# Windowed attention with two gated layers on one core: value loads moved one sequence earlier in the load queue

## The chip, the cores and the metric

The kernel runs on one core of a Trainium2 chip. The metric is the time of the whole program on the device in microseconds (us); three runs of the kernel before gave 895.91, 896.13 and 896.91, a median of 896.13. Lower is better.

## The reference, cut to what matters

The program computes attention in a sliding window of 64 positions (4 batches, 8 heads, 576 positions, head size 64), and feeds its output, 2304 tokens of 512 values, to two layers:

```python
scores = scale * np.matmul(q, k.transpose(0, 1, 3, 2))
mask = (rel >= 0) & (rel < 64)                      # rel = query position - key position
attn = softmax(np.where(mask, scores, -1e9))
x = np.matmul(attn, v)                              # -> (2304, 512)
xn = x / sqrt(mean(x * x) + 1e-6) * rms_g           # layer 1
x = (silu(xn @ w_gate) * (xn @ w_val)) @ w_out      # d_ff 1536
x = square(maximum(x @ w_in, 0)) @ w_out2           # layer 2, d_ff 2048
```

All inputs and outputs are float32.

## The kernel before, in words

Two heads of one batch form a "sequence" of the kernel: there are 16 of them (SEQS), each with 9 blocks of 64 queries. The two heads lie in the two halves of the 128 partitions. q of a sequence is loaded into a block-diagonal tile, `q_diag`, by two transfers of 144 KB (one for each head, L357 and L358); k by one transfer of 288 KB into `k_sb` (L353); v by two transfers of 256 KB, `v_odd` and `v_even` (both L365). All of these are issued by SyncE (SP) on one queue, except three for the first sequence that ScalarE issues at the start (k of sequence 0, and the second head's q of it in two parts). q, k and v each have three buffers (QR, VR).

Four blocks form a group; 36 groups cover the 144 blocks, and a group can straddle two sequences. Every compute engine walks through slots `g` in an order written out by hand. In slot g TensorE computes the scores of group g (L611; where a sequence begins, a matmul with a mask, L606, comes first), then transposes the probabilities of group g-4 (L619), then multiplies the probabilities of group g-5 with v (L631). VectorE picks the window and takes maximum and sum (L1165 to L1180), ScalarE takes the exponential (L936) and copies out of PSUM, GpSimd (POOL) divides and masks (L506, L512). TensorE waits for q and k of a sequence where its first block stands in a group, and for v there five slots later. The first block of sequence s is block 9s, so it stands in group 9s // 4: groups 0, 2, 4, 6, 9, 11, 13, 15, 18, 20, 22 and so on.

The first group's inputs have a semaphore of their own, `first_in` (three transfers: k of sequence 0 and the q of its first four blocks for both heads). SP waits for it before it loads q of sequence 1.

A later load waits for its buffer to come free. q and k of sequence i wait until the scores of the last group that holds blocks of sequence i-3 are done (`qk_done`); v of sequence i waits until the v product of the last group of sequence i-3 is done (`pv_done`). `last_group(s)` is (9s+8)//4: 2, 4, 6, 8, 11, 13, 15 and so on. SP issues its transfers strictly in program order, so a wait for one buffer also holds back everything behind it. Within the loop SP also loads the first weights of layer 1: `load_w` behind the loads of iterations 3 and 5, `load_d` behind those of 8 and 9.

After slot 35 the attention part runs out, mixed with the normalisation of the first tokens and the first products of layer 1; from about 103 us on the two layers run with TensorE as the main engine. Nothing there is touched.

Of the kernel before, what the change touches and what calls it, by code (L numbers as in the profile page):

```python
# [52 lines left out]
SEQS = KT * BATCH  # L53
# [8 lines left out]
QR = 3  # L62
# [4 lines left out]
def last_group(seq):  # L67

    return (seq * NBLK + NBLK - 1) // GU
# [55 lines left out]
def build(nc, qT, kT, v_odd_in, v_even_in, w_gate, w_val, w_out, gains, w_in, w_down, outT):  # L125
    with ExitStack() as ctx:
# [132 lines left out]
        def first_layer(r):  # L259
            return r < PAIRS  # L260

        def tok(r):
            return r % PAIRS * PW
# [12 lines left out]
        def half_cols(r, k, c):  # L276

            return acts[:, k * TOKENS + tok(r) + c * NT:k * TOKENS + tok(r) + (c + 1) * NT]
# [5 lines left out]
        def two(t):  # L284
            return t.rearrange("p (k t) -> p k t", k=2)
# [17 lines left out]
        def steps_done(u):  # L303

            return u + 1 - PLAIN
# [11 lines left out]
        def raw_part(u, n, count=1):  # L317
            return w_raw[u % 2][:, n * HALF_K:(n + count) * HALF_K]
# [18 lines left out]
        def first_rows(row, part):  # L337

            return qT[bass.ds(row, HD), :].rearrange("d (b c) -> d b c", c=WIN)[:, part, :]
# [4 lines left out]
        @block.sync  # L344
        def _(sp):
            def q_rows(row):
                return qT[bass.ds(row, HD), :].rearrange("d (b c) -> d b c", c=WIN)

            def load_k(i):
                par = i % QR  # L350
                if i >= QR:
                    sp.wait_ge(qk_done, last_group(i - QR) + 1)
                sp.dma_start(k_sb[par][:], kT[bass.ds(i * P, P), :]).then_inc(qk_in[par], 16)  # L353

            def load_q(i):
                par = i % QR
                sp.dma_start(q_diag[par][0:WIN, :, 0:WIN], q_rows(i * P)).then_inc(qk_in[par], 16)  # L357
                sp.dma_start(q_diag[par][WIN:P, :, WIN:P], q_rows(i * P + HD)).then_inc(qk_in[par], 16)  # L358

            def load_v(i):  # L360
                n = i % VR
                if i >= VR:
                    sp.wait_ge(pv_done, last_group(i - VR) + 1)
                for dst, src in ((v_odd[n], v_odd_in), (v_even[n], v_even_in)):
                    sp.dma_start(dst[:].rearrange("p m c -> p (m c)"), src[bass.ds(i * P, P), :]).then_inc(v_in[n], 16)  # L365

            def load_w(u):

                if u >= 2:
                    sp.wait_ge(lo1_done, u - 1)  # L370
                    if u - 2 >= PLAIN:
                        sp.wait_ge(s_add, 4 * steps_done(u - 2))
                r = max(n for n in range(RUNS) if U0[n] <= u)
                s = u - U0[r]
                one, two_ = ((w_gate, s), (w_val, s)) if first_layer(r) else ((w_in, 2 * s), (w_in, 2 * s + 1))
                rows = [w.rearrange("(k p) f -> p k f", p=P)[:, :, n * P:(n + 1) * P] for w, n in (one, two_)]
                sp.dma_start(raw_part(u, RAW_A11, 2).rearrange("p (k f) -> p k f", k=KT),
                             rows[0]).then_inc(w_raw_in[u % 2], 16)
                sp.dma_start(two(raw_part(u, RAW_A21)), rows[1][:, 0:2, :]).then_inc(w_raw_in[u % 2], 16)
                if u >= 2:  # L380
                    sp.wait_ge(lo2_done, u - 1)
                sp.dma_start(two(raw_part(u, RAW_A22)), rows[1][:, 2:4, :]).then_inc(w_a22_in[u % 2], 16)

            def load_d(m):

                if m >= 2:
                    sp.wait_ge(dlo_done, m - 1)
                r = max(n for n in range(RUNS) if M0[n] <= m)
                src = w_out if first_layer(r) else w_down
                n = m - M0[r]  # L390
                sp.dma_start(d_raw[m % 2][:], src[n * P:(n + 1) * P, :]).then_inc(d_in_sem[m % 2], 16)

            def store(r, c):
                for k in range(KT):
                    if k % 2 == 0:
                        sp.wait_ge(evac_act, 4 * r + 2 * c + k // 2 + 1)
                    else:
                        sp.wait_ge(evac_dve, 4 * r + 2 * c + k // 2 + 1)
                    to = tok(r) + c * NT
                    sp.dma_start(outT[k * P:(k + 1) * P, to:to + NT], half_cols(r, k, c)).then_inc(stored, 16)  # L400

            sp.dma_start(q_diag[0][0:WIN, 0:GU, 0:WIN], first_rows(0, slice(0, GU))).then_inc(first_in, 16)
            sp.dma_start(q_diag[0][0:WIN, GU:NBLK, 0:WIN], first_rows(0, slice(GU, NBLK))).then_inc(qk_in[0], 16)
            load_k(1)
            sp.wait_ge(first_in, 48)
            load_q(1)
            load_k(2)
            load_q(2)
            load_v(0)
            sp.dma_start(gain[:], gains).then_inc(gain_in, 16)  # L410
            for i in range(SEQS):
                if i + QR < SEQS:
                    load_k(i + QR)
                    load_q(i + QR)
                if i + 1 < SEQS:
                    load_v(i + 1)
                if i in (3, 5):
                    load_w((i - 3) // 2)
                if i in (8, 9):
                    load_d(i - 8)  # L420

            for r in range(RUNS):
                for u in range(U0[r] + (2 if r == 0 else 3), U0[r + 1] + 2):
                    if u < U0[RUNS]:
                        load_w(u)
                for m in range(M0[r] + 2, M0[r + 1] + 2):
                    if m < M0[RUNS]:
                        load_d(m)
                if r + 1 < RUNS:
                    load_w(U0[r + 1] + 2)  # L430
                if not first_layer(r):
                    store(r, 0)
                    store(r, 1)
            sp.wait_ge(stored, 16 * 2 * KT * PAIRS)
# [963 lines left out]
```

## Time and profile before

| what | us |
|---|---|
| median of 3 runs | 896.13 |
| the profiled execution, its own time | 895.91 |
| its span, from first to last instruction | 894.2 |
| TensorE busy in the span | 883.4 |
| POOL busy | 576.1 |
| VectorE busy | 562.1 |
| ScalarE busy | 482.0 |

The execution's own time is 1.7 us more than its span. The kernel has two parts of unlike nature: attention in the first tenth, in which the transfers run nearly all of the time, and the two layers in the rest, in which they run about a fifth of it. The change touches loads of the first part alone.

### The profile page before, as it was taken

The page shows a single profiled execution, that of the slowest core. Times are in us where ns is not written, and L with a number is a line of the kernel's source. Part 1 is how long each engine was busy: PE and PEld are TensorE (multiplying, and loading weights), DVE is VectorE, ACT ScalarE, POOL GpSimd, SP SyncE. Part 2 cuts the span into 40 slices and gives each one's busy share as a digit, 9 for nine tenths or more (in the row PEclk, how much of TensorE's full clock was granted, in tenths as well). Part 3 has the DMA queues.
Part 4 walks back from the last instruction along what each step waited for, and adds up shares of the span by engine and source line. Part 5 has one row for each costly group of instructions (what it writes and reads, how often), then busy time and mean ns, then how long its engine had stood idle before and what let it go on. Part 6 is the DMA issues. An engine that isn't in the chain of part 4 may idle for free.

```text
span 894.2 us, 14547 instructions
## 1 busy us (share of the span) xinstructions
PE 883.4 (99%) x5356; PEld 879.4 (98%) x5356; DVE 562.1 (63%) x735; ACT 482.0 (54%) x848; POOL 576.1 (64%) x539
## 2 busy tenths in 40 slices
PE   7999999999999999999999999999999999999998
PEld 6999999999999999999999999999999999999998
DVE  7687658557757647855556767677377675577222
ACT  3897765635466654455554455544355544455332
POOL 7897579755379757368867368473387653585332
PEclk9999999999999999999999999999999999999999
DMA  9995222112222212222221222222422122420122
GB/s 226 260 254 139 61 71 72 57 57 71 73 75 71 72 54 59 83 66 74 74 72 50 82 63 77 61 60 71 141 78 72 54 61 70 147 71 27 51 71 95
DMA packets 105974, 76.97 MB, mean 86 GB/s; under 512 B 24496, under 2 KB 89008, under 8 KB 105904
## 3 DMA queue, kind: packets, MB, share of 16 engines
q1 hardware_dynamic: 105152, 75.60, 30.6%
q8 instruction: 43, 0.70, 0.4%
q10 hardware_dynamic: 752, 0.44, 0.2%
q14 instruction: 27, 0.22, 0.1%
HBM read 71.31 MB, written 4.72 MB: 85 GB/s over the span
## 4 chain that ended last, share of the span: by engine, by line
PE 94%; POOL 2%; ACT 1%; DVE 1%; issue 0%; DMA 0%; ACTq 0%; POOLq 0%; DVEq 0%
PE bank L656 29%; PE bank L658 29%; PE bank L657 29%; PE bank L611 2%; PE bank L631 2%; POOL wide L512 1%; PE bank L619 1%; POOL probs L506 1%; POOL sq L521 0%; ACT acts L854 0%; PE bank L650 0%; PE bank L641 0%; DMA q_diag<-in_qT 0%; ACT probsT L854 0%; DVE acts L1122 0%
## 5 line engine op out<-in xcount | busy, mean ns | idle before, releaser
L656 PE MATMUL bank<-xc_hi,w_hi 128*128 128x384 f32 x844 | 282.7, 335 | 0.0
L658 PE MATMUL bank<-xc_hi,w_lo 128*128 128x384 f32 x844 | 282.0, 334 | 0.0
L657 PE MATMUL bank<-xc_lo,w_hi 128*128 128x384 f32 x844 | 281.9, 334 | 0.0
L554 POOL TENSOR_TENSOR d_lo<-d_raw,d_hi 128x512 fp32r<-128x512 f32 x84 | 127.3, 1516 | 174.5 <-ACT d_hi L854 174.5
L656 PE MATMUL bank<-hs_hi,d_hi 128*128 128x384 f32 x672 | 225.1, 335 | 0.1
L658 PE MATMUL bank<-hs_hi,d_lo 128*128 128x384 f32 x672 | 224.5, 334 | 0.0
L657 PE MATMUL bank<-hs_lo,d_hi 128*128 128x384 f32 x672 | 224.5, 334 | 0.0
L1255 DVE TENSOR_TENSOR hs_lo<-h,hs_hi 128x768 fp32r<-128x768 f32 x84 | 86.4, 1029 | 137.1 <-ACT hs_hi L854 136.9
L657 PEld LDWEIGHTS bank<-xc_lo,w_hi 128*128 128x128 f32 x844 | 158.5, 188 | 0.0
L656 PEld LDWEIGHTS bank<-xc_hi,w_hi 128*128 128x128 f32 x844 | 158.5, 188 | 0.0
L658 PEld LDWEIGHTS bank<-xc_hi,w_lo 128*128 128x128 f32 x844 | 158.4, 188 | 0.0
L854 ACT ACTIVATE hs_hi<-h 128x768 fp32r<-128x768 f32 x84 | 70.8, 843 | 138.7 <-PE bank L658 138.7
L1099 DVE TENSOR_TENSOR w_lo<-w_raw,w_hi 128x1024 fp32r<-128x1024 f32 (+1 forms) x60 | 82.1, 1368 | 82.2 <-ACT w_hi L854 81.9
L656 PEld LDWEIGHTS bank<-hs_hi,d_hi 128*128 128x128 f32 x672 | 126.1, 188 | 1.4 <-issue 0.7
L657 PEld LDWEIGHTS bank<-hs_lo,d_hi 128*128 128x128 f32 x672 | 126.1, 188 | 0.0
L658 PEld LDWEIGHTS bank<-hs_hi,d_lo 128*128 128x128 f32 x672 | 126.1, 188 | 0.0
L854 ACT ACTIVATE w_hi<-w_raw 128x1024 fp32r<-128x1024 f32 (+1 forms) x120 | 111.7, 931 | 0.0
L478 POOL TENSOR_TENSOR w_raw<-w_raw 128x256 f32<-128x256 f32 x58 | 64.3, 1108 | 40.9 <-DMA w_raw<-in_w_val 22.7
L1108 DVE TENSOR_TENSOR w_lo<-w_raw,w_hi 128x768 fp32r<-128x768 f32 (+1 forms) x60 | 72.8, 1213 | 0.0
L547 POOL TENSOR_TENSOR h<-sbb,vb 128x384 f32<-128x384 f32 x34 | 55.7, 1637 | 25.1 <-ACT sbb L979 25.0
L985 ACT ACTIVATE sa<-ga 128x384 f32<-128x384 f32 x58 | 30.5, 526 | 66.0 <-DVE ga L1276 65.8
L854 ACT ACTIVATE c_t<-bank 128x384 f32<-128x384 f32 x58 | 28.5, 492 | 65.3 <-PE bank L658 65.3
(90 smaller groups left out, 1199.3 us busy)
## 6 DMA issues: line engine op xcount, KB each, us to landing
d_raw<-in_w_down SPq DMA_DIRECT2D x48, 256.0 KB, 2.6
w_raw<-in_w_gate SPq DMA_DIRECT2D x36, 256.0 KB, 2.9
w_raw<-in_w_val SPq DMA_DIRECT2D x72, 128.0 KB, 2.8
d_raw<-in_w_out SPq DMA_DIRECT2D x36, 256.0 KB, 2.6
w_raw<-in_w_in SPq DMA_DIRECT2D x24, 256.0 KB, 2.7
w_raw<-in_w_in SPq DMA_DIRECT2D x48, 128.0 KB, 2.5
out_T<-acts SPq DMA_DIRECT2D x24, 192.0 KB, 3.0
k_sb<-in_kT SPq DMA_DIRECT2D x15, 288.0 KB, 4.7
```

The source lines that it names most:

```text
L478: nc.gpsimd.tensor_tensor(raw_part(u, RAW_S3), raw_part(u, RAW_A11), raw_part(u, RAW_A21), ALU.subtract).then_inc(s_add, 1)
L547: nc.gpsimd.tensor_tensor(h_half(n, 1), sbuf_b[:], vb[:], ALU.mult).then_inc(hb_done, 1)
L554: nc.gpsimd.tensor_tensor(d_lo[m % 2][:], d_raw[m % 2][:], d_hi[m % 2][:].bitcast(F32), ALU.subtract).then_inc(dlo_done, 1)
L611: mm = pe.matmul(ps, q_diag[par][:, b, :], keys, start=b > 0, stop=True)
L656: pe.matmul(ps, w_h, v_h, start=first, stop=False, skip_group_check=joined)
L657: pe.matmul(ps, w_h, v_l, start=False, stop=False, skip_group_check=joined)
L658: return pe.matmul(ps, w_l, v_h, start=False, stop=last, skip_group_check=joined)
L854: nc.scalar.activation(to, of, ACT.Copy).then_inc(done, 1)
L985: nc.scalar.activation(sa[:], ga[:], ACT.Silu if first_layer(r) else ACT.Relu).then_inc(act_a_done, 1)
L1099: nc.vector.tensor_tensor(w_lo[u % 2][:, to], w_raw[u % 2][:, of], w_hi[u % 2][:, to].bitcast(F32), ALU.subtract).then_inc(lo1_done, 1)
L1108: nc.vector.tensor_tensor(w_lo[u % 2][:, to], w_raw[u % 2][:, of], w_hi[u % 2][:, to].bitcast(F32), ALU.subtract).then_inc(lo2_done, 1)
L1255: nc.vector.tensor_tensor(hs_lo[m % 2][:], h_chunk(r, m - M0[r]), hs_hi[m % 2][:].bitcast(F32), ALU.subtract).then_inc(hlo_done, 1)
```

## The change

In the prologue the k load of sequence 1 is issued behind the wait for `first_in` instead of ahead of it; v of sequence 1 is loaded right behind v of sequence 0, and q and k of sequence 2 come behind both. In the loop, iteration i loads v of sequence i+2 where it loaded v of sequence i+1. The k and q loads of one sequence, two helper functions before, are one. The same transfers are made as before.

```diff
-            def load_k(i):
+            def load_qk(i):
                 par = i % QR
                 if i >= QR:
                     sp.wait_ge(qk_done, last_group(i - QR) + 1)
                 sp.dma_start(k_sb[par][:], kT[bass.ds(i * P, P), :]).then_inc(qk_in[par], 16)
-
-            def load_q(i):
-                par = i % QR
                 sp.dma_start(q_diag[par][0:WIN, :, 0:WIN], q_rows(i * P)).then_inc(qk_in[par], 16)
                 sp.dma_start(q_diag[par][WIN:P, :, WIN:P], q_rows(i * P + HD)).then_inc(qk_in[par], 16)
...
-            load_k(1)
             sp.wait_ge(first_in, 48)
-            load_q(1)
-            load_k(2)
-            load_q(2)
+            load_qk(1)
             load_v(0)
+            load_v(1)
+            load_qk(2)
             sp.dma_start(gain[:], gains).then_inc(gain_in, 16)
             for i in range(SEQS):
                 if i + QR < SEQS:
-                    load_k(i + QR)
-                    load_q(i + QR)
-                if i + 1 < SEQS:
-                    load_v(i + 1)
+                    load_qk(i + QR)
+                if i + 2 < SEQS:
+                    load_v(i + 2)
                 if i in (3, 5):
                     load_w((i - 3) // 2)
                 if i in (8, 9):
```

## Rows read from the trace of the kernel before

**Rows 1.** Windows: stretch, us, busy time (count) of each engine, granted clock, DMA share, GB/s
```profile
12.00:66.00 54.00, 53.92 (x482) 53.23 (x482) 41.06 (x127) 45.29 (x117) 47.68 (x54) 1.00 1.16 261
66.00:103.00 37.00, 35.10 (x287) 34.16 (x286) 24.32 (x62) 30.36 (x71) 30.14 (x32) 1.00 0.44 116
103.00:894.00 791.00, 788.09 (x4558) 786.44 (x4556) 488.64 (x529) 403.92 (x659) 490.96 (x426) 1.00 0.24 71
```
**Rows 2.** Waits, 0 to 13 us: waiter <- awaited: us in total, times, longest us
```profile
PE bank L606 <- DMA q_diag<-in_qT: 4.7, 1, 4.7
PEld bank L606 <- DMA q_diag<-in_qT: 0.3, 1, 0.3
```
**Rows 3.** Waits, 13 to 46 us, the longest in total
```profile
DVE bank L1165 <- PE bank L611: 8.9, 13, 0.8
```
**Rows 4.** Timeline of SP, 0 to 21 us: start us, us, queue, line, what is issued
```profile
2.25 0.61 SPq L353 DMA_DIRECT2D k_sb<-in_kT  x1
...
4.67 0.55 SPq L357 DMA_DIRECT2D q_diag<-in_qT  x1
5.25 0.64 SPq L358 DMA_DIRECT2D q_diag<-in_qT  x1
...
7.86 0.62 SPq L365 DMA_DIRECT2D v_odd<-in_v_odd  x1
8.52 0.43 SPq L365 DMA_DIRECT2D v_even<-in_v_even  x1
...
20.50 0.33 SPq L365 DMA_DIRECT2D v_odd<-in_v_odd  x1
```
**Rows 5.** Timeline of TensorE: where sequences 1, 2, 5, 7, 9 begin (L606), two v products
```profile
8.96 0.23 PE L606 MATMUL bank<-first_mask,ident_bf 128*128 128x128 bf16 x1
...
12.27 0.22 PE L606 MATMUL bank<-first_mask,ident_bf 128*128 128x128 bf16 x1
...
27.30 0.22 PE L606 MATMUL bank<-first_mask,ident_bf 128*128 128x128 bf16 x1
...
29.19 0.39 PE L631 MATMUL bank<-probsT,v_odd 128*128 128x128 f32 x2
...
36.86 0.22 PE L606 MATMUL bank<-first_mask,ident_bf 128*128 128x128 bf16 x1
...
40.52 0.39 PE L631 MATMUL bank<-probsT,v_even 128*128 128x128 f32 x2
...
47.75 0.22 PE L606 MATMUL bank<-first_mask,ident_bf 128*128 128x128 bf16 x1
```
**Rows 6.** Line L358 (second half of q), the issues at 5.25 and 7.18 us
```profile
L358 SPq DMA_DIRECT2D q_diag<-in_qT x2: 635/636/637, 5.3 to 7.2; - x2
...
DMA to landing us min/median/max: 3.7/4.2/4.8
```
**Rows 7.** Line L365 (v), the issues at 7.86 and 8.52 us
```profile
L365 SPq DMA_DIRECT2D v_even<-in_v_even x1: 432/432/432, 8.5 to 8.5; - x1
...
DMA to landing us min/median/max: 4.5/4.6/4.7
```
**Rows 8.** Line L358, the issues at 10.90 and 13.97 us
```profile
L358 SPq DMA_DIRECT2D q_diag<-in_qT x2: 635/635/635, 10.9 to 14.0; - x2
...
DMA to landing us min/median/max: 5.2/5.7/6.2
```
**Rows 9.** Line L358, the issues at 22.41 and 29.24 us
```profile
L358 SPq DMA_DIRECT2D q_diag<-in_qT x2: 637/1134/1631, 22.4 to 29.2; - x2
...
DMA to landing us min/median/max: 6.5/6.8/7.1
```
**Rows 10.** Line L358, the issues at 33.79 and 40.04 us
```profile
L358 SPq DMA_DIRECT2D q_diag<-in_qT x2: 935/1150/1366, 33.8 to 40.0; - x2
...
DMA to landing us min/median/max: 6.7/6.8/6.9
```
**Rows 11.** Timeline of TensorE: scores of groups 0 and 1, then of group 8
```profile
4.80 3.33 PE L611 MATMUL bank<-k_sb,q_diag 128*128 128x128 f32 x16
...
20.30 1.06 PE L611 MATMUL bank<-k_sb,q_diag 128*128 128x128 f32 x8
```

## The prediction, made before the changed kernel ran

> **What bounds the kernel now.** I read the windows first. TensorE is busy 53.92 of the 54 us between 12 and 66, 35.10 of 37 in the rest of attention, and 788.09 of 791 in the two layers [rows 1]. The change reaches only loads of the first part, so it acts by moving the moment at which that part ends; the layers then follow at their own pace. In 12 to 66 there is no idle time on TensorE worth 0.1 us that an earlier transfer could remove, while any wait put in there is passed on whole. At the same time the transfers run at 261 GB/s with a DMA share of 1.16, against 116 and 71 GB/s later [rows 1]: the queue is full, and what is moved ahead pushes something else back.
>
> Then the waits. TensorE waits for a transfer 4.7 us at the start (the first q) and 0.3 us at sequence 1 [rows 2]. From 13 to 46 us no wait for a transfer is listed at all; the longest in total is VectorE's for the scores [rows 3]. No engine waits for v anywhere. So the change brings forward transfers for which nobody waits.
>
> Last, how much room q and k have, from issue and landing. The two q issues of rows 6 land at 5.25 + 3.7 = 8.95 and 7.18 + 4.8 = 11.98; TensorE begins sequences 1 and 2 at 8.96 and 12.27 [rows 5]. Sequence 1 is just in time, sequence 2 has 0.3 us. Later ones: sequence 7 lands at 29.24 + 6.5 = 35.74 [rows 9] and is used at 36.86 [rows 5], 1.1 us of room; sequence 9 lands at 40.04 + 6.9 = 46.94 [rows 10] for use at 47.75, 0.8 us of room. Sequence 5 is used at 27.30.
>
> **The price of a transfer in the full queue.** q of sequences 3 and 4 land at 10.90 + 5.2 = 16.10 and 13.97 + 6.2 = 20.17 [rows 8], so k, q and v of one sequence, 1088 KB, take 4.07 us. v of sequence 0 lands at 8.52 + 4.7 = 13.22 [rows 7], 1.24 us after q of sequence 2 and 2.88 us before q of sequence 3. I take 1.3 us for v of one sequence and 2.8 us for its k and q.
>
> **Step 1, sequence 1.** Before, its k was issued at 2.25 and its q from 4.67 on [rows 4]. Now k is issued at 4.67, behind `first_in`. A k issue takes 0.33 to 0.61 us and the first q half 0.55 [rows 4] (0.33 is what the first issue behind a wait takes there), so the second half is issued at 5.6 to 5.9 instead of 5.25. With the same 3.7 us it lands at 9.3 to 9.6; I take 9.5. That is 0.5 us late.
>
> **Step 2, sequence 2: the largest term.** Behind it now stand v of sequences 0 and 1 and then k and q of sequence 2. The queue needs 1.3 + 1.3 + 2.8 = 5.4 us for them, so q of sequence 2 lands at 14.9. The issues give nearly the same: 5.75 + 0.64 for q, twice 0.62 + 0.43 for v [rows 4], 0.61 and 0.55, with some 0.04 between issues, put the last q issue at 9.8, and with its 4.8 us [rows 6] it lands at 14.6. TensorE needs it at 12.27. The wait of step 1 lies inside this one, since both end on the same queue, so the two are not added: 14.9 - 12.27 = 2.6 us of lateness, from which I take 0.1 for the slots 4 and 5, where TensorE no longer waits for VectorE. 2.5 us. Ends: with the fastest second half of the rows, 3.7 us, it lands at 13.5, 1.2 us late; with a slower queue at 15.4, 3.1 us late.
> The Trainium skill, page "DMA: Bandwidth & Descriptors", section "Bandwidth", gives about 358 GB/s as what one core gets from HBM. By that, an estimate, the 1600 KB of v0, v1, k2 and q2 would take 4.6 us instead of 5.4 and the lateness would be 1.8 instead of 2.6. The trace has 261 GB/s in the full queue [rows 1], so I stay with the rows.
>
> **Step 3, the loop.** v of sequence i+2 now waits for the v product of the last group of sequence i-1, slot last_group(i-1) + 5, and k and q of sequence i+4 stand behind it on SP. Before, SP stood at v of sequence i+1, free three to four slots earlier. Example: v of sequence 3 was issued at 20.50 [rows 4], when the v product of group 2 was done. q and k of sequence 5 were issued ahead of that; now they stand behind it. With 2.5 us of lateness that is 23.0, when the queue has already run dry (q of sequence 2 at 14.9, sequence 3 and v2 by 19.0, sequence 4 by 21.8). From empty: an issue-to-landing of about 4.1 us for v (nearest row: 4.5 to 4.7 [rows 7]) and 2.8 behind it, 29.9. Used at 27.30 + 2.5 = 29.8: 0.1 us late.
> Sequence 6: v4 is issued at about 27.6, k and q behind it; queue 29.9 + 4.1 to 5.3 (sequence 6 landed at 22.41 + 7.1 = 29.51 before [rows 9]) = 34.0 to 35.2, just about when it is wanted: 0 to 0.4 late. I put 0.2 for 5 and 6 together.
> Sequence 7: v5 waits for group 6's v product, which ended at 29.58 [rows 5], so 32.2 now. Behind it come v5, the weights of `load_w(0)` (512 KB) and k, q of 7. From q6 to q7 the queue took 35.74 - 29.51 = 6.2 us before, with the same load between. From 34.0 to 35.2 it is 40.2 to 41.4, and wanted at 36.86 + 2.7 = 39.6: 0.6 to 1.8 late; lower if it is issued into a less full queue. I take 0.9.
> Sequence 8 has `load_w` behind it and over a microsecond of room: nothing.
> Sequence 9: v7 waits for group 11's v product, end 40.91 [rows 5] plus 3.6 = 44.5. The queue before took 46.94 - 40.49 = 6.45 us from q8 (33.79 + 6.7 [rows 10]) to q9; q8 now lands at about 45, q9 at 51.5 to 52.4, wanted at 47.75 + 3.6 = 51.35: 0.2 to 1.2 late. I take 0.7.
> After that slots take as long or longer and only `load_d`, half a `load_w`, stands between: nothing more.
>
> **What is passed on.** TensorE has 0.08 us idle in 12 to 66, so all of it arrives at 66. In 66 to 103 it has 1.9 us idle [rows 1], in waits for ScalarE and POOL, which themselves shift with the scores; I let 0.2 be taken back. The layers start so much later and cost the same.
> Gains from the change: v lands sooner, for which nobody waits: 0. `first_in` may come earlier, since k of sequence 1 no longer shares the queue with it. It came at 4.65 while the last of its transfers issued on SP needs no more than about 3 us; 0 to 0.5 us, and SP moves with it. I count 0.
>
> **Sum.** 2.5 + 0.2 + 0.9 + 0.7 - 0.2 = 4.1 us on the profiled execution's 895.91: 900.0. That execution lies 0.2 below the median of the runs, so I say 900.2.
>
> **The rivals.**
> (a) Only the start waits. The later room absorbs the order in the loop, because the queue, once behind, is less full and lands sooner than 6.5 us. For it: landings of 3.7 and 4.8 in the emptier queue [rows 6] against 6.5 to 7.1 in the full one [rows 9]. Against it: in 5, 6, 7 and 9 the sum rests on bytes and issue times, not on the depth of the queue. 895.9 + 2.5 - 0.2 = 898.3.
> (b) Not slower: the issue order does not decide when bytes move. With `first_in` 0.5 us earlier and all of SP with it, and the q of sequence 2 landing 3.0 us after an issue at 9.3, sequence 2 is there at 12.3, when it is wanted. It decides from a landing before about 12.3 on, and is worth 0 to -0.5 us: 895.7. Against it: no second half of q landed in less than 3.7 us [rows 6], and 1 MB more stands ahead of it.
> (c) The clock. The granted clock is 1.00 in all windows [rows 1], yet the scores of groups 0 and 1, right after the initial wait, took 3.33 us for 16 matmuls, where 8 take 1.06 later [rows 11]; 1.2 us more than warm. If a wait of 2 us at sequence 2 brings that back once, the time is 900.2 + 1.2 = 901.4, and twice 902.6. Against it: between 8 and 12 us TensorE already waits several times and runs at the later pace.
> The Trainium skill, page "TensorE: Matmul & The Clock Gate", section "HAM oscillation — how this bites in real kernels", says that waits for transfers let the gate fall back to half rate and the next matmuls start slow. That is this rival; the rows of this kernel show it only after the initial wait.
> (d) The loop's order costs more than I allow: the v wait makes each round from v product to q landing the pace, and sequences 8, 10 or 11 wait too, some 0.5 us each. 902 to 903.
>
> **Chances.** Forecast 0.60, (a) 0.17, (b) 0.06, (c) 0.07, (d) 0.10. What a measurement of this kernel can tell from no change is about 0.2%, 1.8 us, so slower means above 897.9. (a) is at 898.3 and a third of it lies below that, with (b) and a small part of the forecast: same 0.14; faster by 1.8 us has no mechanism but an error of mine: 0.03; slower 0.83. The range of 8 in 10 goes from 897.8 (the low end of step 2 with little in the loop) to 903.0 (3.1 at the start, 1.8 and 1.2 in the loop, and a part of (c) or (d)).
>
> **What would show it.** Right: a wait of PE L606 for a q or k transfer of over 1 us near 12.8 to 15, in the waits of 0 to 16 us; SP's v issue at about 23 ahead of k of sequence 5; short waits of TensorE for transfers before sequences 7 and 9; L606 of sequence 9 at about 51.9; layers as long as before (788 us busy in 791). The mean rate in 12 to 66 falls below 261 GB/s. Wrong: if sequence 2 begins before 13; if the wait is there and the attention part still ends at 103; or if waits for transfers appear at sequences 10 and later.

## The result, and the profile after

The changed kernel takes 905.97 us (median; 903.09 to 906.0), the kernel before 896.13. The ratio is 1.0099 with a 95% interval of 1.0082 to 1.0116: 9.8 us slower (7.3 to 10.4 by the interval). The forecast was 900.2, with a range of 897.8 to 903.0. The direction was right; the 4.1 us of the forecast are less than half of the loss, and the measured time lies 3 us above the range. The profiled execution took 906.16 us with a span of 904.4, so 10.2 us more span than before; it is this one that is taken apart here. (One more execution of it took 1162.92 us at a mean granted clock of 0.71 and is left out of all numbers.)

The windows of the changed kernel, in the columns of [rows 1]:

```profile
12.00:66.00 54.00, 46.53 (x391) 45.49 (x391) 34.63 (x108) 35.71 (x92) 38.51 (x44) 0.97 0.83 202
33.00:34.00 1.00, 1.00 (x11) 1.00 (x10) 0.32 (x1) 0.87 (x3) 0.83 (x2) 1.00 0.20 43
34.00:43.40 9.40, 6.52 (x59) 6.31 (x57) 4.63 (x15) 5.71 (x15) 6.12 (x7) 1.00 0.98 250
44.00:50.00 6.00, 6.00 (x42) 6.00 (x41) 3.08 (x10) 3.74 (x10) 3.51 (x5) 0.72 0.27 46
66.00:103.00 37.00, 36.26 (x317) 35.72 (x317) 27.27 (x81) 31.69 (x76) 30.81 (x34) 1.00 0.67 194
113.00:904.00 791.00, 788.36 (x4559) 786.71 (x4558) 489.68 (x529) 404.17 (x660) 491.14 (x426) 1.00 0.24 71
```

The layers are as before (788.36 us busy in 791, against 788.09 [rows 1]). TensorE, which had 0.08 us idle in 12 to 66, now has 7.5. The transfers (the last two columns: DMA share, the mean busy share of the core's 16 transfer engines, and GB/s) fell from 261 to 202 GB/s, and in 44 to 50, where before they ran at about 247, to 46 GB/s. In the same six microseconds the granted clock is 0.72: for part of them TensorE ran at half clock, 1.2 instead of 2.4 GHz. Before that it had waited 2.93 us for q of sequence 7, and had then worked for about 0.9 us when the clock fell.

The waits of the changed kernel, 0 to 110 us, the two that answer to [rows 2] (the first-block matmul is on L601 now):

```profile
PEld bank L601 <- DMA q_diag<-in_qT: 9.5, 5, 3.1
PE bank L601 <- DMA q_diag<-in_qT: 8.4, 4, 2.9
```

And where TensorE begins sequences 1, 2, 5, 7, 8 and 9, from its timeline (against [rows 5]):

```profile
9.87 0.29 PE L601 MATMUL bank<-first_mask,ident_bf 128*128 128x128 bf16 x1 [0.94 <-DMA q_diag<-in_qT]
...
15.83 0.23 PE L601 MATMUL bank<-first_mask,ident_bf 128*128 128x128 bf16 x1 [1.74 <-DMA q_diag<-in_qT]
...
30.79 0.23 PE L601 MATMUL bank<-first_mask,ident_bf 128*128 128x128 bf16 x1
...
43.45 0.23 PE L601 MATMUL bank<-first_mask,ident_bf 128*128 128x128 bf16 x1 [2.93 <-DMA q_diag<-in_qT]
...
51.20 0.22 PE L601 MATMUL bank<-first_mask,ident_bf 128*128 128x128 bf16 x1
...
58.93 0.23 PE L601 MATMUL bank<-first_mask,ident_bf 128*128 128x128 bf16 x1 [2.79 <-DMA q_diag<-in_qT]
```

The lateness grows in four jumps. It is 3.56 us at sequence 2 (15.83 - 12.27), 3.31 at 3, 3.50 at 6, 6.59 at 7 (43.45 - 36.86), 8.23 at 8 (51.20 against 42.97), 11.18 at 9 (58.93 - 47.75), and then shrinks to 10.23 at sequence 13 and stays there to the end. The jump from 7 to 8 has no wait in it: it is the half clock, in which eight matmuls of the scores took 1.91 us where the next eight took 1.06:

```profile
45.84 1.91 PE L606 MATMUL bank<-k_sb,q_diag 128*128 128x128 f32 x8
...
48.98 1.06 PE L606 MATMUL bank<-k_sb,q_diag 128*128 128x128 f32 x8
```

SP's timeline shows why 7 and 9 wait (v on L362, second half of q on L355):

```profile
28.36 0.33 SPq L362 DMA_DIRECT2D v_odd<-in_v_odd  x1
...
30.27 0.64 SPq L355 DMA_DIRECT2D q_diag<-in_qT  x1
...
33.10 0.33 SPq L362 DMA_DIRECT2D v_odd<-in_v_odd  x1
...
36.59 0.64 SPq L355 DMA_DIRECT2D q_diag<-in_qT  x1
37.66 0.75 SPq L362 DMA_DIRECT2D v_odd<-in_v_odd  x1
...
40.93 0.64 SPq L355 DMA_DIRECT2D q_diag<-in_qT  x1
...
49.17 0.33 SPq L362 DMA_DIRECT2D v_odd<-in_v_odd  x1
...
52.65 0.64 SPq L355 DMA_DIRECT2D q_diag<-in_qT  x1
```

The landings of the q issues at 36.59 and at 52.65 us, then of the v issue at 37.66:

```profile
DMA to landing us min/median/max: 6.8/6.8/6.8
...
DMA to landing us min/median/max: 6.2/6.2/6.2
...
DMA to landing us min/median/max: 5.4/5.4/5.4
```

Each q now belongs to a **round**: a v buffer is released, v goes out, weights if any, then k and q. The round's length is from the v issue to q's landing; its room is from the same release to the first use of q, which is TensorE's own work. From before: room for sequence 5 is 27.30 - 20.50 = 6.8, for 7 36.86 - 29.58 = 7.3, for 9 47.75 - 40.91 = 6.8 [rows 4, 5]. Rounds in the changed kernel: sequence 5 (no weights) 23.80 to 30.77, 7.0 us, just in time for its use at 30.79. Sequence 6 (no weights) 28.36 to 34.17, 5.8 us, no wait. Sequence 7, with 512 KB of weights, 33.10 to 36.59 + 6.8 = 43.39: 10.3 us, 3.0 over the room; the wait is 2.93. Sequence 9, with weights, 49.17 to 52.65 + 6.2 = 58.85: 9.7 us, 2.9 over; the wait is 2.79. Between 41.6 and 49.2 SP issues nothing: it stands at v of sequence 7, whose release TensorE, late itself, holds back.

That round minus room gives the wait is nearly an identity, since both are read from the same landing. What has to be explained is why the rounds with weights are so long. Their own bytes do not account for it: v, weights, k and q of sequence 7 are 1600 KB, 1.64 MB, which at the 261 GB/s of [rows 1] would take 6.3 us. Two things in the windows and issues above make up the rest. The queue had run empty before the round (share 0.20 in 33 to 34). And transfers issued behind q moved before q had landed: from 34.0 to 43.4 the queue carried 250 GB/s, 2.35 MB, 0.7 MB more than the round holds, and the first half of v of sequence 6, issued at 37.66, landed at 43.06, ahead of q's 43.39. Here transfers are issued in order and do not land in order. The round of 9 is alike (2.4 MB, and v's first half issued at 53.73 landed at 58.33, ahead of q).

### The profile page after: what moved, and what is told of

Same layout as the page of the kernel before. It is cut to its first block, busy times and chain, and to the rows that moved or that the text cites. A ratio compares the mean times of both kernels' runs of the same rounds, so it can differ in the third digit from the quotient of the medians.

```text
span 904.4 us, 14547 instructions
## 1 busy us (share of the span) xinstructions
PE 886.7 (98%) x5356; PEld 882.9 (98%) x5356; DVE 563.0 (62%) x735; ACT 482.1 (53%) x848; POOL 575.9 (64%) x539
## 4 chain that ended last, share of the span: by engine, by line
PE 94%; DMA 3%; SPq 1%; ACT 1%; DVE 1%; issue 0%; ACTq 0%
PE bank L651 29%; PE bank L653 29%; PE bank L652 29%; DMA q_diag<-in_qT 3%; PE bank L626 2%; PE bank L606 2%; PE bank L614 1%; ACT acts L849 0%; PE bank L645 0%; PE bank L636 0%; SPq L362 0%; ACT probsT L849 0%; DVE acts L1117 0%; SPq L354 0%; SPq L353 0%
## 5 line engine op out<-in xcount | busy, mean ns | idle before, releaser
L473 POOL TENSOR_TENSOR w_raw<-w_raw 128x256 f32<-128x256 f32 x58 | 63.2, 1090 | 41.6 <-DMA w_raw<-in_w_val 22.6
```

The costliest lines, as they stand in the source:

```text
L473: nc.gpsimd.tensor_tensor(raw_part(u, RAW_S3), raw_part(u, RAW_A11), raw_part(u, RAW_A21), ALU.subtract).then_inc(s_add, 1)
```

## The experiments

Each ran beside the kernel before; its median there was 896.25 (e1 to e4), 896.26 (e5 to e8) and 896.46 (e9 to e12). The mean granted clock of an execution tells how much of it ran at half clock: 1.000 is none, and the lower, the more. Among the executions with a trace, 0.998 is one stretch (the changed kernel, e10), 0.996 also one, about twice as long (e3, e9, e11), and 0.994 a long and a short one (e2). Waits and landings below are those of the one execution with a trace. A single trace carries about half a microsecond of play: with the same prologue, sequence 2 began at 15.38 to 15.88 in seven traces (the changed kernel, e1, e3, e5, e6, e9, e11).

**e1: the prologue alone**

```diff
-                if i + 2 < SEQS:
-                    load_v(i + 2)
+                if 0 < i and i + 1 < SEQS:
+                    load_v(i + 1)
```

> Only the prologue of the change; in the loop v is loaded as before, one sequence ahead. Theory A (two separate prices: the issue order at the start costs 3.3 us, the wait for a v buffer ahead of q and k in the loop costs the other 6.9 us): TensorE waits at sequences 1 and 2, none at 7 and 9, sequence 9 begins near 51.1, total 899 to 900. Theory B (one price: the late start alone drains the queue's lead, the loop's order is harmless): waits at 7 and 9 of 2 to 3 us as in the changed kernel, total 904 to 906.

Measured: 899.62, ratio 1.0044 (1.0028 to 1.0061). Sequence 2 begins at 15.38, 7 at 39.72, 9 at 50.61, neither with a wait: 3.1 us late at sequence 2, 2.9 from sequence 3 on, and 2.8 in the span. By clock: 898.78 and 898.94 at 1.000, 900.3 and 901.45 at 0.998.

```profile
15.38 0.23 PE L601 MATMUL bank<-first_mask,ident_bf 128*128 128x128 bf16 x1 [1.42 <-DMA q_diag<-in_qT]
...
39.72 0.22 PE L601 MATMUL bank<-first_mask,ident_bf 128*128 128x128 bf16 x1
...
50.61 0.22 PE L601 MATMUL bank<-first_mask,ident_bf 128*128 128x128 bf16 x1
```

Theory A holds, B falls: lateness from the start does not breed waits by itself.

**e2: the loop alone** (the prologue of before; iteration 0 also loads v of sequence 1)

```diff
-                if i + 1 < SEQS:
-                    load_v(i + 1)
+                if i == 0:
+                    load_v(1)
+                if i + 2 < SEQS:
+                    load_v(i + 2)
```

> Only the loop of the change (v two sequences ahead, its second load added in iteration 0); prologue as before. Theory A: sequence 2 begins at 12.3 as before, but q of 5, 7 and 9 stand behind the v wait: waits of TensorE at 7 and 9 of 2.5 to 3 us each, perhaps 1.6 us of half clock, total 900.5 to 903. Theory B: 896 to 897 with no wait for a transfer after 13 us.

Measured: 902.02, ratio 1.0065 (1.004 to 1.0089). In the profiled execution, the slowest with 905.63, TensorE waits at 7 and at 9 as in the changed kernel, with two stretches of half clock (0.994), one from the wait at 7 on, which made the way to sequence 8 2.7 us longer than before, one behind the wait at 9, 1.5 us. A wait of 0.49 us at sequence 13 comes on top.

```profile
12.99 0.22 PE L608 MATMUL bank<-first_mask,ident_bf 128*128 128x128 bf16 x1
...
41.01 0.29 PE L608 MATMUL bank<-first_mask,ident_bf 128*128 128x128 bf16 x1 [3.22 <-DMA q_diag<-in_qT]
...
56.80 0.23 PE L608 MATMUL bank<-first_mask,ident_bf 128*128 128x128 bf16 x1 [2.04 <-DMA q_diag<-in_qT]
```

At full clock it took 898.93 and 900.2. So the loop costs 2.7 to 4 us without half clock and 5.8 at the median. The losses of e1 and e2 at the median, 3.4 and 5.8, add up to 9.1 of the 9.8.

**e3: a fourth v buffer in the changed kernel**

```diff
-VR = 3
+VR = 4
...
+        v_odd.append(sb("v_odd3", [P, NBLK // 2, P], F32, temp_at))
+        v_even.append(sb("v_even3", [P, NBLK // 2, P], F32, temp_at + NBLK // 2 * P * 4))
```

> The changed kernel with a fourth v buffer (laid over temporaries that attention does not use), so that v of sequence i+2 waits for the v product of sequence i-2, done two slots earlier than the wait of the changed kernel; the order of all transfers is that of the changed kernel. Theory A (the wait is what costs in the loop): the waits at 7 and 9 go, the start's 3.3 us stay, 899 to 900. Rival C (the order costs: v and weights ahead of q and k in the queue, whenever they are issued): waits at 7 and 9 remain above 2 us, 904 to 906.

Measured: 900.09, ratio 1.0042 (1.0028 to 1.0056); 898.34 and 898.57 at clock 1.000. No wait at 7 or 9. The profiled execution (901.69, span 900.0) fell to half clock during the wait for sequence 2: its granted clock in 12 to 20 was

```profile
12.00:20.00 8.00, 5.17 (x26) 4.98 (x26) 4.05 (x13) 1.85 (x4) 5.15 (x6) 0.65 1.12 262
```

and its timeline around it

```profile
15.54 0.29 PE L603 MATMUL bank<-first_mask,ident_bf 128*128 128x128 bf16 x1 [2.44 <-DMA q_diag<-in_qT]
...
17.43 1.91 PE L608 MATMUL bank<-k_sb,q_diag 128*128 128x128 f32 x8
...
22.12 0.22 PE L603 MATMUL bank<-first_mask,ident_bf 128*128 128x128 bf16 x1
```

From sequence 2 to 3 it took 6.58 us instead of 4.14 [rows 5 for 12.27; 16.41 before]. Order of transfers unchanged, wait gone, loop loss gone: it is the wait, not the order. Rival C falls.

**e4: k of sequence 1 ahead of the wait again, in the changed kernel**

```diff
+            sp.dma_start(k_sb[1][:], kT[P:2 * P, :]).then_inc(qk_in[1], 16)
             sp.wait_ge(first_in, 48)
-            load_qk(1)
```

(with the two q transfers of sequence 1 behind the wait)

> The changed kernel with k of sequence 1 issued ahead of the wait for first_in, as before. Theory D (two v ahead of q of sequence 2 make its lateness): sequence 1 begins near 9.0 instead of 9.9, sequence 2 at 14.9 to 15.4 instead of 15.8, total 904.8 to 905.6. Theory E (k of sequence 1 behind first_in makes it): sequence 2 begins by 13, total 902 to 903.

Measured: 903.86, ratio 1.0092 (1.0068 to 1.0116), as slow as the changed kernel within the interval. Its start is better: sequence 1 at 9.13, sequence 2 at

```profile
14.60 0.23 PE L603 MATMUL bank<-first_mask,ident_bf 128*128 128x128 bf16 x1 [1.70 <-DMA q_diag<-in_qT]
```

although its first scores began 0.25 us later than before (4.99). So putting k back ahead gains 1.2 us at sequence 2, and 2.3 us of lateness are left with the two v. Sequence 2 begins between what D and E said (14.9 to 15.4, or by 13), nearer to D.

**e5: the weights ahead of v in iterations 3 and 5 of the changed kernel**

```diff
-                if i + 2 < SEQS:
-                    load_v(i + 2)
                 if i in (3, 5):
                     load_w((i - 3) // 2)
+                if i + 2 < SEQS:
+                    load_v(i + 2)
```

> The changed kernel with the weight loads of iterations 3 and 5 issued ahead of the v of the same iteration instead of behind it. Theory F (the waits at 7 and 9 arise because v, 512 KB of weights, k and q must all pass between the release of a v buffer and the use of q; without weights in it the round is about 5.8 us, as for sequence 6, and fits): no wait at 7 and 9, only the start's 3.3 us, 899 to 900.5. Rival G (the v wait alone makes the round too long, whatever stands in it): waits at 7 and 9 stay at 1.5 us or more, 902 to 905.

Measured: 902.69, ratio 1.0071 (1.0056 to 1.0086); 901.23 at clock 1.000. The wait at 9 is gone, that at 7 is halved (and there are short ones at 5, 0.34, and at 13, 0.48):

```profile
42.18 0.23 PE L601 MATMUL bank<-first_mask,ident_bf 128*128 128x128 bf16 x1 [1.46 <-DMA q_diag<-in_qT]
```

The round of 7 ran from v's issue at 33.30 to 42.12, 8.8 us, 1.5 over the room of 7.3: the weights, issued only just before, were still in the queue. F in part, G in part; the two were not cleanly apart here.

**e6: filler matmuls ahead of the waits of the changed kernel**

```diff
+                            for _ in range({2: 24, 7: 44, 9: 44}.get(seq, 0)):
+                                pe.matmul(bank[0][:, 0:P], ident_bf[:], first_mask[:], start=True, stop=True)
                             if seq > 0:
                                 pe.wait_ge(qk_in[par], ...)
```

> The changed kernel with 24, 44 and 44 small matmuls into a bank that nobody reads then, ahead of the waits for q at sequences 2, 7 and 9, so that TensorE works on while it would wait (about 1.3, 2.4 and 2.4 us of work in waits of 1.7, 2.9 and 2.8). Theory H (a wait of that length sometimes brings the half clock, which costs about 1.6 us each and spreads the runs): the arrival times of q stay, granted clock 1.00 in all stretches, the runs lie closer together, median 1 to 2 us below the changed kernel, near 904. Rival (the spread has another cause): same median and spread.

Measured: 904.4, ratio 1.0092 (1.0077 to 1.0107). The filler of sequence 7 and the matmul behind it:

```profile
39.74 2.62 PE L598 MATMUL bank<-first_mask,ident_bf 128*128 128x128 bf16 x44
42.20 0.22 PE L603 MATMUL bank<-first_mask,ident_bf 128*128 128x128 bf16 x1
```

Three of four executions stayed at clock 1.000 (903.03, 904.91, 906.05), the fourth at 0.998 (903.89); all five of the changed kernel's counted executions had 0.998. So filling the wait mostly keeps the clock. The median is 1.6 us lower, near the 904 expected, but the two kernels' executions overlap over nearly their whole ranges, so this gain is not shown. The spread of 3 us stayed: it comes from elsewhere too, and the expectation is half met. The filler itself also ran 0.4 us past q's landing at 41.78. What moves the landings by a microsecond or two between executions was not found.

**e7: the kernel before, with only k of sequence 1 behind the wait**

```diff
-            load_k(1)
             sp.wait_ge(first_in, 48)
+            load_k(1)
```

> The kernel before with only the k of sequence 1 moved behind the wait for first_in. Theory D (two v ahead of q of sequence 2 make most of the start's lateness): sequence 1 begins 0.5 to 0.9 us late, sequence 2 by 13.2, total 896.5 to 897.2. Theory E (k of sequence 1 makes most): sequence 2 near 14.5 or later, total above 898.

Measured: 897.80, ratio 1.0016 (1.0006 to 1.0026). Sequence 1 begins at

```profile
10.60 0.29 PE L606 MATMUL bank<-first_mask,ident_bf 128*128 128x128 bf16 x1 [1.66 <-DMA q_diag<-in_qT]
...
14.48 0.22 PE L606 MATMUL bank<-first_mask,ident_bf 128*128 128x128 bf16 x1
```

1.64 us late, where I expected 0.5 to 0.9, and sequence 2 with no wait of its own 2.2 late. The issue of q at 5.47 landed after 5.1 us, against 3.7 [rows 6]: before, k was issued 3.0 us ahead of q, now 1.0 us ahead, so its 288 KB are still under way beside q's. Sequence 2 is where E had it, and the total lies between the two. Set against e4, this means that the parts do not add: k alone makes sequence 2 2.2 us late here, and the two v without k 2.3 there, where both together make 3.56.

**e8: the kernel before, with only v of sequence 0 ahead of k and q of sequence 2**

```diff
             load_q(1)
+            load_v(0)
             load_k(2)
             load_q(2)
-            load_v(0)
```

> The kernel before with only v of sequence 0 moved ahead of k and q of sequence 2. Theory D: 1.1 to 1.3 us of transfer stand ahead of q of sequence 2, it lands near 13.1 to 13.4 instead of 12.0, TensorE begins sequence 2 about 1 us late, total 897 to 897.6. Theory E: under 0.4 us late, within noise of the kernel before.

Measured: 896.96, ratio 1.0006 (0.9996 to 1.0015): no change. Sequence 2 begins at

```profile
12.38 0.22 PE L606 MATMUL bank<-first_mask,ident_bf 128*128 128x128 bf16 x1
```

0.1 us late, E's side again. q of sequence 2 landed at 7.89 + 4.4 = 12.29, 0.3 later than before (11.98), and that uses up the 0.3 us of room that it had. The queue is not full yet at that point (DMA share 0.81 in 4.5 to 8 us, against 1.16 later), so the first v delays q little. By difference, 2.2 of e4's 2.3 us would be the second v's; no run moves that one alone, so this split is argued. D's 1.3 us for each v does not hold for the first.

**e9: both weight loads in iteration 1 of the changed kernel**

```diff
+                if i == 1:
+                    load_w(0)
+                    load_w(1)
                 if i + 2 < SEQS:
                     load_v(i + 2)
-                if i in (3, 5):
-                    load_w((i - 3) // 2)
```

> The changed kernel with both weight loads of the loop issued in iteration 1, ahead of v of sequence 3, where the changed kernel's queue ran dry (17.5 to 23.8 us). Theory F (1 MB of weights inside two rounds between v release and use of q makes the waits at 7 and 9): no wait at 7 and 9, at most 0.5 us at 5 and 7; 899 to 900.5 at full clock, and 1.6 us more where a run has one spell of half clock. Rival G (the v wait alone makes the rounds too long): over 1.5 us at 7 again, 902 to 904.

Measured: 901.49, ratio 1.005 (1.0034 to 1.0066); 898.65 at clock 1.000, 901.41 and 901.58 at 0.998, 902.1 at 0.996. Sequences 7 and 9 begin without a wait:

```profile
43.02 0.22 PE L602 MATMUL bank<-first_mask,ident_bf 128*128 128x128 bf16 x1
...
53.91 0.22 PE L602 MATMUL bank<-first_mask,ident_bf 128*128 128x128 bf16 x1
```

The round of 7 is 35.77 to 42.38, 6.6 us, and fits its 7.3. F holds, G falls. The profiled execution lost 2.6 us to half clock at sequence 2 instead, as in e3, and waited 0.49 us at sequence 10.

**e10: the same with the prologue of before and the loop of the change**

> Prologue of before, loop of the change, both weight loads in iteration 1. Theory F: no wait for a transfer after 13 us except small ones, 896 to 897. Rival G: 1 to 3 us of waits at 7 and 9, 898.5 to 902.

Its edit is that of e9, made in e2. Measured: 901.00, ratio 1.0052 (1.0037 to 1.0067). A miss: 896 to 897 was expected. 7 and 9 do not wait, but 5 does:

```profile
31.85 0.29 PE L609 MATMUL bank<-first_mask,ident_bf 128*128 128x128 bf16 x1 [3.60 <-DMA q_diag<-in_qT]
...
42.73 0.22 PE L609 MATMUL bank<-first_mask,ident_bf 128*128 128x128 bf16 x1
```

With a timely start the queue is not dry in iteration 1. The megabyte of weights took SP until 23.97 to issue and stood ahead of v of 3 and k and q of 5. Its v buffer was free at about 21.2, q landed at 31.76: a round of 10.5 us in a room of 6.8, 3.7 too long, 3.60 waited. Half clock from the wait on made the way to sequence 6 another 1.3 us longer. Moving the weights moves the wait to the round that they stand in.

**e11: only the first weight load in iteration 1 of the changed kernel**

```diff
+                if i == 1:
+                    load_w(0)
...
-                if i in (3, 5):
-                    load_w((i - 3) // 2)
+                if i == 5:
+                    load_w(1)
```

> The changed kernel with only the first weight load moved to iteration 1; the second stays in iteration 5. Theory I (the wait at 9 has its own cause, the second weight load in its round): no wait at 7, 2 to 3 us at 9, 901.5 to 903.5. Theory J (the wait at 9 follows from that at 7, which held up v of 7 and so what stands behind it): no wait at 7 and under 1 us at 9, 899 to 900.5.

Measured: 903.61, ratio 1.008 (1.0062 to 1.0098), none of its executions at full clock. Sequence 5 waits 0.74 us (a round of 7.7 in a room of 6.8), 7 does not, and at 9

```profile
56.19 0.23 PE L603 MATMUL bank<-first_mask,ident_bf 128*128 128x128 bf16 x1 [1.43 <-DMA q_diag<-in_qT]
```

Its round, 47.80 to 56.18, is 8.4 us, 1.5 over the room. So 9 has its own cause (I), though 1.43 is below I's 2 to 3 us. It is half the changed kernel's wait. Whether the other half comes from the wait at 7 or from the spread of landings stays open; that spread is large enough: the rounds of 7 and 9 with their weights, left as in the change, take 9.3 to 10.6 us and 9.0 to 10.2 us in the traces of the changed kernel, e2, e4 and e6. Here v's first half behind q landed at 56.65, after q, and the round carried 2.1 MB instead of 2.4.

**e12: the prologue of before, the loop of the change, a fourth v buffer**

> Prologue of before, loop of the change, a fourth v buffer. Theory A (the loop's order is free once v need not wait for the product of sequence i-1): as the kernel before, 896 to 896.8, no wait for a transfer after 13 us. Rival C (the order costs by itself): 898 or more.

Its edit is that of e3, made in e2. Measured: 896.82 over 10 executions, ratio 1.0005 (0.9995 to 1.0015): as the kernel before. One short wait is left, at 7, where none was expected:

```profile
38.09 0.23 PE L610 MATMUL bank<-first_mask,ident_bf 128*128 128x128 bf16 x1 [0.60 <-DMA q_diag<-in_qT]
```

A holds: v two sequences ahead is free if its load need not wait. It gains nothing either. No variant was faster than the kernel before.

## Why the prediction was right or wrong

- **Mechanism and sign: right.** No engine waited for v, and the waits came where q was pushed back, at sequences 1, 2, 7 and 9, as forecast; the layers were untouched. The forecast missed 6.1 of 10.2 us, mostly by the size of three terms: 0.8 at sequence 2, 2.2 at 7, 2.3 at 9, and 1.6 for the clock, less 0.75 that were taken back beyond the 0.2.
- **Step 1 (0.5 us): mis-sized.** 0.91 in the profile, 1.64 alone in e7. I took 3.7 us from issue to landing from a q whose k had been issued 3.0 us ahead; behind a k issued 1 us ahead it is 4.4 in the changed kernel and 5.1 in e7.
- **Step 2 (2.5 us): 3.3 after the slots that give 0.25 back.** From q of 1 to q of 2 the queue took 5.9 us (9.86 to 15.80), not 5.4, and it began 0.4 late by step 1. My prices per transfer, 1.3 us for 512 KB of v and 2.8 for 576 KB of k and q, were split from one pair of landings; used for two v and one k and q they imply 303 GB/s. The mean rate of [rows 1], 261 GB/s, which I named as my reason to stay with the rows, gives 6.3 us for the same 1600 KB. The queue moved at 265 GB/s there, so that rate was the better price, and the one with which my price should have been compared.
- **Step 3, sequences 5 and 6 (0.2): right**, 3.31 to 3.50. (The text says that SP's wait moved three to four slots; by `last_group` it is two or three. No term used it.)
- **Step 3, sequence 7 (0.9): the step that failed, 3.1.** I let v5, weights, k and q follow sequence 6 without a gap, "6.2 us" after it had landed. Sequence 6 landed at 34.17, as forecast (34.0 to 35.2), but 7 came 9.2 us after it, not 6.2. v5 waits for its buffer (issued at 33.10), and the queue ran empty meanwhile, as in the windows above. The 6.2 us is an interval between two landings in a queue that never empties: by the first of them, part of the next load has already moved (before, the first half of v4 landed at 29.15, ahead of q6's 29.51). From an empty queue nothing has, and the round also carried 0.7 MB of what was issued behind it. So the time is to be counted from the v release. A row near to that was there to be read before:

```profile
25.05 0.33 SPq L365 DMA_DIRECT2D v_odd<-in_v_odd  x1
```

From this v4 to q7's landing at 35.74 it is 10.7 us with the same load between, and 10.3 were measured. That they are so close is in part luck, since the 10.7 hold the rest of sequence 6's load, too, and 10.3 hold the restart of the queue. Against the room of 7.3 it would have given about 3.
- **Step 3, sequence 9 (0.7): the same error, 2.95** (9.7 in a room of 6.8). That the v wait makes the loss is shown by e3 and e12, in which it goes with the wait. That the weights in the rounds make them too long is shown by e9, which takes them out and removes both waits, and by e10, which puts them into the round of 5 and moves the wait there. That what is issued behind q lengthens them too is read from the traces; no run was made to separate it.
- **The clock (rival c, 0.07): 1.6 us missing from the sum.** It came on top of the forecast, not in its place. All five counted executions of the changed kernel had some half clock (0.998); that the longer waits brought it is argued from e6. I had put it in a rival of small chance, for the reason that TensorE ran at its later pace after short waits. The Trainium skill, page "TensorE: Matmul & The Clock Gate", section "HAM oscillation — how this bites in real kernels", says that waits for transfers bring half rate; the traces agree, with 1.6 us lost after a wait of 2.93 and 2.4 after one of 2.44 (e3). It is no certainty: after the wait of 2.79 at sequence 9 the clock stayed full, and after one of 3.22 in e4.
- **What is passed on (0.2 taken back): 0.95**, between sequences 9 and 13, so nearly 5 times as much. That it is TensorE's small gaps there, filled by work that had piled up, is argued, not tested.
- Sum: 3.31 + 0.19 + 3.09 + 1.64 + 2.95 - 0.95 = 10.23, the difference of the spans.
- **Rival (d)** named the right thing, the round from v product to q landing, but placed it at 8, 10 or 11 and priced it at 0.5 us. The long rounds are those with weights in them.

## What to carry to other kernels

When a load is moved ahead of others on an in-order queue and waits for a buffer, write down for each transfer behind it two numbers: the length of the round from that release to its landing, and the compute between the release and its use. A wait appears where the first is larger, and the heaviest round decides, not the mean rate: here 5.8 us fitted and 10.3 did not. Intervals between landings in a queue that was full before tell little once the new wait lets it run dry, and what is issued right behind a transfer can still delay its landing. Prefetching v, for which nobody waited, gained nothing in any run here and cost time in most. If such a prefetch is wanted, give it one more buffer: that took the loop's loss from 5.8 us (e2) to none clear of noise (e12).

## What the runs showed of the hardware that I had not expected

- A wait of TensorE of 2 to 3.6 us is followed by half clock in some executions and not in others: 2.04 at 9 in e2 was, 2.04 at 7 in e4 was not; 3.22 at 7 in e2 was, 3.22 at 9 in e4 was not. A stretch of it cost 1.3 (e10) to 2.7 us (e2). The clock can fall during the wait (e3) or after it (the changed kernel). The executions of the kernels with such waits spread over 1 to 7 us, those of the kernel before over 0.4 to 1.4.
- The same 512 KB of v cost 0.1 us at one place of the start (e8), and by difference about 2.2 at the next (e4): the queue's share of time was 0.81 at the first, and q had 0.3 us of room there.
- Transfers of one queue are issued in order and can land out of order: v's first half, issued 1.07 us behind q's last, landed 0.33 us before it (the changed kernel, sequence 7).
- From an empty queue, v's first half landed 2.5 to 2.8 us after its issue (the changed kernel from 23.80 us on); in the full one of the kernel before it took 4.1 to 6.0.
